# Attention in front of two expert stages: load order, the sink copy, four weight subtractions and the mask steps moved

## Chip, core and metric

The kernel runs on one core of a Trainium2 chip. The metric is the device time of one execution in microseconds. Two things have to be kept apart: the time of a run, and the span of one profiled execution, which is a little shorter than that execution's own time.

## What is computed

Inputs are `q`, `k`, `v` of shape (2, 8, 768, 64), batch by heads by tokens by head size. Three stages follow each other.

```python
scores = q @ k.T / sqrt(D)                       # per batch and head
keep = (key < n_sink) | ((row - key >= 0) & (row - key < window))   # n_sink 4, window 128
a = softmax(where(keep, scores, -1e9))
x = (a @ v)                                      # to 1536 tokens x 512
g = x @ w_gate;  x = (silu(g) * (x @ w_val)) @ w_out               # d_ff 1536
# then each token with skip_score > 0 goes to the one of 8 experts with the largest logit:
out = x + gate * relu(x @ w1[e]) @ w2[e]         # d_ff 1024
```

## The kernel before

**Attention.** The 1536 tokens are 12 tiles of 128 rows (`NT`), 6 for each batch (`QT`). Each tile has 4 pairs of heads (`HP`), so there are 48 pairs in all, numbered n. A row sees only its own tile, the tile before it and the sinks, so a tile other than the first of its batch has 208 score columns per head, of which 16 are a copy of the batch's first 16 keys, kept beside each key tile in `k_sb`. The first tile of a batch has 128 columns, and less work.

One list, `ORDER`, made by `attention_order()` (line 55), fixes the order of steps on TensorE, VectorE and ScalarE alike. It goes by groups g = 0, 2, 4, and so on. In group g each engine takes these steps, as far as they are its own:

- S for pairs g and g+1: TensorE makes scores (lines 1138 and 1145), VectorE adds the mask and finds the maximum (line 839), ScalarE takes the exponential (line 614)
- X for a finished tile: VectorE scales the tile's output into `xT` (line 862)
- T for pairs g-3 and g-2: TensorE transposes the probabilities (line 1166), VectorE (line 847) or, for the last pair of a tile, ScalarE (line 622) copies them from PSUM to `probsT`. With a tile's last pair goes Q: VectorE makes the reciprocals of the sums (lines 851 and 854)
- V for pairs g-5 and g-4: TensorE multiplies by the values (lines 1181, 1189). With a tile's last pair goes R: GpSimd spreads the reciprocals (line 526), TensorE transposes them (line 1159), ScalarE copies them (line 628)
- K, two mask steps on VectorE (`make_mask`, line 802, instructions of line 807). K for mask 1 comes right behind S of pair 2, K for mask 0 right behind S of pair 5 together with `find_wide` (lines 812 to 818). Mask 1 is first used in group 4, mask 0 in group 8
- W and M for the tiles in `EARLY` (7 to 10): at pair 1 of the tile ScalarE rounds a quarter of the next stage's first weights into `w_hi` (line 603); at pair 2, in the same group, VectorE subtracts to get `w_lo` (line 823)

TensorE's S of a group waits until the maxima of two groups of banks earlier are made (line 1134), and its second and later T until the copy of the T two before it is made (line 1155).

**Loads.** All of attention's loads are issued by SyncE (lines 358 to 382), in one queue: for each tile the columns of q and k (lines 367 and 368), then the values (lines 374 to 377). Columns of the second batch overwrite those of the first and wait for scores long made. From tile 3 on the values wait until the V steps of the tile three before are done (line 372), and everything issued later stands behind that wait. Between the tiles of batch 0 and those of batch 1 come five loads of weights (lines 380 to 382, 1554 KB together).

**GpSimd.** Its loop over tiles (lines 517 to 530) copies the sinks into the key tiles at tiles 0 and 6 (line 523), spreads the reciprocals of the tile, and then splits the tile before into `x_hi` and `x_lo` (lines 511 and 514). TensorE's first S of tiles 1 and 7 waits for the sink copy (line 1131).

**Behind attention** TensorE runs slices of the dense stage (lines 1198 to 1216): slice f needs 2f+2 halves of `w_lo`, its first chunk 8 split tiles, its last all 12. SyncE's next weight loads wait for `w_lo` too (line 399).

Of the kernel before, what the change touches and what calls it, by code (L numbers as in the profile page):

```python
# [7 lines left out]
F32 = mybir.dt.float32  # L8
# [6 lines left out]
P = 128  # L15
B, H, S, D = 2, 8, 768, 64
DM = H * D
QT = S // P
NT = B * QT
HP = H // 2  # L20
SK = 16
# [3 lines left out]
TAIL = SC - P  # L25
SINKS = slice(P, KT)
# [15 lines left out]
KB = 1024  # L42
PAIRS = NT * HP
EARLY = range(NT - 5, NT - 1)
MASK_AT = {2: 1, 5: 0}
TURNED = 4
WARM_UP = 24

# [6 lines left out]
def attention_order():  # L55

    steps, psum_use, turned = [], 0, {}  # L60
    for g in range(0, PAIRS + 10, 2):
        for n in (g, g + 1):
            if n < PAIRS:
                steps.append(("S", n // HP, n % HP, n))
                if n in MASK_AT:
                    steps.append(("K", MASK_AT[n], None, n))
        for n in (g - 7, g - 6):
            if 0 <= n < PAIRS and n % HP == HP - 1:
                steps.append(("X", n // HP, None, n // HP))
        for n in (g - 3, g - 2):  # L70
            if 0 <= n < PAIRS:
                steps.append(("T", n // HP, n % HP, psum_use))
                turned[psum_use] = n
                psum_use += 1
                if n % HP == HP - 1:
                    steps.append(("Q", n // HP, None, n // HP))
        for n in (g - 5, g - 4):
            if 0 <= n < PAIRS:
                tile, hp = divmod(n, HP)
                steps.append(("V", tile, hp, None))  # L80
                if hp == HP - 1:
                    steps.append(("R", tile, None, psum_use))
                    psum_use += 1
                if tile in EARLY and hp in (1, 2):
                    steps.append(("W" if hp == 1 else "M", tile, None, tile - EARLY[0]))
    v_use = itertools.count()
    return [(k, t, h, next(v_use)) if k == "V" else (k, t, h, n) for k, t, h, n in steps], turned

# [3 lines left out]
LAST_V = {tile: use for kind, tile, _, use in ORDER if kind == "V"}  # L92
# [10 lines left out]
def build(nc, qT, kT, v, va, vb, sizes, w_gv, w_out, w_route, w1, w2, out):  # L103
    ctx = ExitStack()
    with ctx:
# [17 lines left out]
        q_sb = place("q_sb", (P, HP, S), 0, 0)  # L123
        k_sb = place("k_sb", (P, HP, QT, KT), 0, 12)
# [231 lines left out]
        @block.sync  # L356
        def _(sp):
            sp.dma_start(sizes_i[:, :], sizes.broadcast_to([P, 4])).then_inc(sizes_in, 16)
            for b in range(B):
                for t in range(QT):  # L360
                    tok = slice(t * P, t * P + P)
                    if b:

                        sp.wait_ge(scores_ready, H * min(t + 2, QT))

                        sp.wait_ge(ksink_made, 1)
                    sp.dma_start(q_sb[:, :, tok], qT[b, :, :, tok]).then_inc(qk_in[t], 16)
                    sp.dma_start(k_sb[:, :, t, 0:P], kT[b, :, :, tok]).then_inc(qk_in[t], 16)
                    tile = b * QT + t
                    if tile >= 3:  # L370

                        sp.wait_ge(pv_done, LAST_V[tile - 3] + 1)
                    if t == 0:
                        sp.dma_start(va_sb[:, tile % 3, 0, :], v[b, 0, :, :]).then_inc(v_in[t], 16)
                    else:
                        sp.dma_start(va_sb[:, tile % 3, :, :], va[b, t - 1, :, :, :]).then_inc(v_in[t], 16)
                        sp.dma_start(vb_sb[0:TAIL, tile % 3, :, :], vb[b, t - 1, :, :, :]).then_inc(v_in[t], 16)
                if b == 0:
                    for f in range(2):
                        sp.dma_start(w_raw[:, f, :, :, :], w_gv[f, :, :, :, :]).then_inc(w_in[f], 16)  # L380
                        sp.dma_start(wo_raw[:, f, :], w_out[f, :, :]).then_inc(wo_in[f], 16)
                    sp.dma_start(wr_sb[:, :, :], w_route).then_inc(wr_in, 16)
# [83 lines left out]
        def _(pool):  # L466
# [41 lines left out]
            def split_x(tile):  # L508
                at_tok = slice(tile * P, tile * P + P)
                pool.wait_ge(o_ready, tile + 1)  # L510
                nc.gpsimd.tensor_copy(x_hi[:, :, at_tok], xT[:, tile % 2, :].rearrange("p (k t) -> p k t", k=KD)
                                      ).then_inc(x_hi_made, 1)
                pool.wait_ge(x_hi_made, tile + 1)
                nc.gpsimd.tensor_tensor(x_lo[:, :, at_tok], xT[:, tile % 2, :].rearrange("p (k t) -> p k t", k=KD),
                                        x_hi[:, :, at_tok].bitcast(F32), ALU.subtract).then_inc(xT_ready, 1)

            for tile in range(NT):
                if tile % QT == 0:

                    pool.wait_ge(qk_in[0], 32 * (tile // QT) + 32)  # L520
                    if tile:
                        pool.wait_ge(scores_ready, QT * H)
                    nc.gpsimd.tensor_copy(k_sb[:, :, 0:QT - 1, SINKS], k_sb[:, :, 0:1, 0:SK].broadcast_to(
                        [P, HP, QT - 1, SK])).then_inc(ksink_made, 1)
                pool.wait_ge(rsum_ready, tile + 1)
                nc.gpsimd.tensor_copy(rsum_wide.rearrange("p (h c) -> p h c", h=H),
                                      rsum[:, tile % 2, :].unsqueeze(2).broadcast_to([P, H, D])).then_inc(rsum_spread, 1)
                if tile:
                    split_x(tile - 1)
            split_x(NT - 1)  # L530

            with pool.Fori(0, FT1 // 2) as j:
# [234 lines left out]
        def _(d):  # L767
# [60 lines left out]
            for kind, tile, h, n in ORDER:  # L828
                qt = tile % QT
                if kind == "S":  # L830
                    cols = slice(0, SC if qt else P)
                    for u in range(2):
                        i = n * 2 + u
                        d.wait_ge(scores_ready, i + 1)
                        if i >= 4:

                            d.wait_ge(probs_ready, i - 3)

                        nc.vector.tensor_tensor_reduce(  # L839
                            out=scores_sb[:, i % 4, cols], in0=scores_ps[i % 4][:, cols],  # L840
                            in1=mask[:, max(2 - qt, 0), cols], scale=SCALE, scalar=3e38, op0=ALU.add, op1=ALU.min,
                            accum_out=negmax[:, i % 4:i % 4 + 1]).then_inc(max_ready, 1)
                elif kind == "T" and not on_act(kind, h):
                    d.wait_ge(pT_in_psum, n + 1)
                    if SBUF_USE[n] >= TURNED:
                        d.wait_ge(pv_done, SBUF_USE[n] - TURNED + 1)
                    nc.vector.tensor_copy(turned(probsT[:, SBUF_USE[n] % TURNED, :], qt), turned(pT_ps[n % 2][:, :], qt)
                                          ).then_inc(pT_by_dve, 1)
                elif kind == "Q":
                    d.wait_ge(probs_ready, tile * H + H)  # L850
                    nc.vector.tensor_scalar(rsum[:, tile % 2, :], sums[:, qt % 2, :], 1e-9, None, ALU.add
                                            ).then_inc(sums_step, 1)
                    d.wait_ge(sums_step, tile + 1)
                    nc.vector.reciprocal(rsum[:, tile % 2, :], rsum[:, tile % 2, :]).then_inc(rsum_ready, 1)
                elif kind == "X":
                    use = next(m for k, t, _, m in ORDER if k == "R" and t == tile)
                    d.wait_ge(pv_done, LAST_V[tile] + 1)
                    d.wait_ge(pT_by_act, evacuated(use)[1])
                    if tile >= 2:

                        d.wait_ge(xT_ready, tile - 1)
                    nc.vector.tensor_tensor(xT[:, tile % 2, :], o_ps[tile % 2][:, :], rbc_sb, ALU.mult
                                            ).then_inc(o_ready, 1)
                elif kind == "M":
                    split_half(n // 2, n % 2, n + 1)
                elif kind == "K":
                    make_mask(tile)
                    if tile == 0:
                        find_wide()
# [69 lines left out]
                        val_ps[(u + c) % 2][:, :].rearrange("p (t c) -> p t c", c=P), ALU.mult).then_inc(h_ready, 1)  # L939

            slice_of_h(0, 0)
            with d.Fori(0, FT1 // 2 - 1) as j:
                for u in (1, 0):
                    f = j * 2 + 2 - u
                    for half in range(2):
                        split_half(1 - u, half, (f + 1) * 2 + half + 1)
                    slice_of_h(f, u)
# [476 lines left out]
```

## Time and profile before

| | us |
|---|---|
| median of 3 runs | 592.85 |
| lowest, highest | 591.88, 593.5 |
| the profiled execution's own time | 595.78 |
| its span | 593.9 |
| attention within it, up to the dense stage's first product | 98.5 |

TensorE is busy for 548.1 us of the span, VectorE for 242.5, ScalarE for 180.7, GpSimd for 92.7. The span starts with the first instruction. The profile draws it in 40 slices of 14.85 us each; attention is the first six and a half. A slice shows busy time in tenths, and the clock that TensorE was granted, also in tenths: full speed is 2.4 GHz, half speed 1.2 GHz. TensorE's busy time is not work done: at half clock the same work is busy for longer.

### The profile page before, as it was taken

The page shows a single profiled execution, that of the slowest core. Times are in us where ns is not written, and L with a number is a line of the kernel's source. Part 1 is how long each engine was busy: PE and PEld are TensorE (multiplying, and loading weights), DVE is VectorE, ACT ScalarE, POOL GpSimd, SP SyncE. Part 2 cuts the span into 40 slices and gives each one's busy share as a digit, 9 for nine tenths or more (in the row PEclk, how much of TensorE's full clock was granted, in tenths as well). Part 3 has the DMA queues.
Part 4 walks back from the last instruction along what each step waited for, and adds up shares of the span by engine and source line. Part 5 has one row for each costly group of instructions (what it writes and reads, how often), then busy time and mean ns, then how long its engine had stood idle before and what let it go on. Part 6 is the DMA issues. An engine that isn't in the chain of part 4 may idle for free.

```text
span 593.9 us, 10567 instructions
## 1 busy us (share of the span) xinstructions
PE 548.1 (92%) x3752; PEld 462.9 (78%) x3752; DVE 242.5 (41%) x675; ACT 180.7 (30%) x419; POOL 92.7 (16%) x132
## 2 busy tenths in 40 slices
PE   6987889999999999999889999999269998999994
PEld 5766667788888888888768888888269997999993
DVE  6874774323333333232223344633624244145411
ACT  4764774110111111111123334321304133144210
POOL 2242335411111100100000110011100111102111
PEclk9997999999999999999979999999669999999998
DMA  8784750211111111000070112761455587755111
GB/s 224 216 266 110 216 157 4 73 53 53 53 53 53 53 53 53 0 0 1 0 284 35 53 53 76 279 230 58 156 172 218 196 313 300 307 212 190 59 36 35
DMA packets 29509, 73.55 MB, mean 124 GB/s; under 512 B 2816, under 2 KB 15104, under 8 KB 25376
## 3 DMA queue, kind: packets, MB, share of 16 engines
q1 hardware_dynamic: 26592, 63.61, 31.1%
q0 software_dynamic: 2880, 9.47, 4.7%
q8 instruction: 22, 0.36, 0.2%
q14 instruction: 15, 0.12, 0.1%
HBM read 61.77 MB, written 11.29 MB: 123 GB/s over the span
## 4 chain that ended last, share of the span: by engine, by line
PE 82%; DMA 7%; DVE 4%; ACT 3%; issue 3%; SPq 1%; POOL 0%; DVEq 0%; POOLq 0%; ACTq 0%
PE bank L1362 11%; PE bank L1203 11%; PE bank L1207 11%; PE bank L1205 11%; PE bank L1277 6%; PE bank L1281 5%; PE bank L1279 5%; PE bank L1374 3%; PE bank L1376 3%; PE bank L1375 3%; PE bank L1189 3%; DMA k_sb<-kT 2%; DMA w_raw<-w 2%; PE bank L1166 2%; PE bank L1145 2%
## 5 line engine op out<-in xcount | busy, mean ns | idle before, releaser
L1203 PE MATMUL bank<-x_hi,w_hi 128*128 128x512 f32 x288 | 112.2, 390 | 0.3 <-issue 0.3
L1207 PE MATMUL bank<-x_hi,w_lo 128*128 128x512 f32 x288 | 112.1, 389 | 0.0
L1205 PE MATMUL bank<-x_lo,w_hi 128*128 128x512 f32 x288 | 112.0, 389 | 0.0
L1362 PEld LDWEIGHTS bank<-xgT,w_sb 128*128 128x128 f32 x704 | 82.8, 197 | 1.9 <-issue 1.2
L1362 PE MATMUL bank<-xgT,w_sb 128*128 128x128 f32 x704 | 83.1, 280 | 0.8 <-ACT xgT L736 0.8
L934 DVE TENSOR_TENSOR sig<-sig,bank 128x512 f32<-128x512 f32 x36 | 24.8, 688 | 131.1 <-ACT sig L656 131.1
L656 ACT ACTIVATE sig<-bank 128x512 f32<-128x512 f32 x36 | 21.5, 599 | 162.6 <-PE bank L1207 162.6
L1277 PE MATMUL bank<-wo_hi,hh_hi 128*128 128x512 f32 x144 | 59.5, 414 | 4.3 <-DVE hh_lo L954 4.3
L1203 PEld LDWEIGHTS bank<-x_hi,w_hi 128*128 128x128 f32 x288 | 54.1, 188 | 11.8 <-issue 0.7
L1205 PEld LDWEIGHTS bank<-x_lo,w_hi 128*128 128x128 f32 x288 | 54.1, 188 | 11.3
L1207 PEld LDWEIGHTS bank<-x_hi,w_lo 128*128 128x128 f32 x288 | 54.0, 188 | 11.2
L1281 PE MATMUL bank<-wo_hi,hh_lo 128*128 128x512 f32 x144 | 57.4, 399 | 0.0
L1279 PE MATMUL bank<-wo_lo,hh_hi 128*128 128x512 f32 x144 | 57.2, 397 | 0.0
L1012 DVE TENSOR_TENSOR w_lo<-w_raw,w_hi 128x1024 fp32r<-128x1024 f32 x32 | 37.3, 1220 | 35.4 <-ACT w_hi L699 35.3
L614 ACT ACTIVATE probs<-scores_sb,negmax 128x208 f32<-128x208 f32 (+1 forms) x96 | 42.8, 448 | 28.1 <-DVE negmax L839 28.1
L699 ACT ACTIVATE w_hi<-w_raw 128x1024 fp32r<-128x1024 f32 x32 | 31.5, 1048 | 32.8 <-PE bank L1376 25.0
L549 POOL DMA_INDIRECT expert_rows<-x,row_i x12 | 11.8, 980 | 174.1 <-DVE row_i L1004 171.1
L839 DVE CUSTOM_DVE_ANT_0 scores_sb<-bank,mask 128x208 f32<-128x208 f32 (+1 forms) x96 | 28.9, 357 | 23.1 <-PE bank L1145 17.3
L1374 PE MATMUL bank<-w_hi,hg_hi 128*128 128x512 f32 x88 | 35.4, 402 | 2.1 <-DVE hg_lo L1092 2.1
L1277 PEld LDWEIGHTS bank<-wo_hi,hh_hi 128*128 128x128 f32 x144 | 27.7, 193 | 9.8 <-issue 4.7
L1376 PE MATMUL bank<-w_hi,hg_lo 128*128 128x512 f32 x88 | 34.4, 391 | 0.0
L1375 PE MATMUL bank<-w_lo,hg_hi 128*128 128x512 f32 x88 | 34.3, 390 | 0.0
(139 smaller groups left out, 692.9 us busy)
## 6 DMA issues: line engine op xcount, KB each, us to landing
w_sb<-w SPq DMA_DIRECT2D x16, 1024.0 KB, 6.2
w_raw<-w SPq DMA_DIRECT2D x16, 1024.0 KB, 9.4
w_raw<-w_gv SPq DMA_DIRECT2D x12, 512.0 KB, 3.6
va_sb<-v_long SPq DMA_DIRECT2D x10, 512.0 KB, 3.5
xg<-expert_rows POOLq DMA_DIRECT2D x13, 257.0 KB
vb_sb<-v_tail SPq DMA_DIRECT2D x10, 320.0 KB, 4.7
q_sb<-qT SPq DMA_DIRECT2D x12, 256.0 KB, 4.8
k_sb<-kT SPq DMA_DIRECT2D x12, 256.0 KB, 5.0
```

The lines of the kernel that those rows point to most:

```text
L614: nc.scalar.activation(probs[:, qt % 2, h * 2 + u, cols], scores_sb[:, i % 4, cols], ACT.Exp, bias=negmax[:, i % 4:i % 4 + 1], scale=-1.0, ...
L1012: last = nc.vector.tensor_tensor(w2_lo[u][:, f:f + FT2 // 4, :].rearrange("p k c -> p (k c)"), w2_raw[:, p, q:q + FT2 // 4, :].rearrange(" ...
L1203: nc.tensor.matmul(ps[:, :], w_hi[:, u, a, k, :], x_hi[:, k, tok], start=(k == 0), stop=False)
L1205: nc.tensor.matmul(ps[:, :], w_hi[:, u, a, k, :], x_lo[:, k, tok], start=False, stop=False)
L1207: last = nc.tensor.matmul(ps[:, :], w_lo[:, u, a, k, :], x_hi[:, k, tok], start=False, stop=(k == KD - 1))
L1277: nc.tensor.matmul(out_ps[u][:, :], hh_hi[:, u, f, :], wo_hi[:, f, :], start=(f == 0), stop=False, skip_group_check=True)
L1279: nc.tensor.matmul(out_ps[u][:, :], hh_hi[:, u, f, :], wo_lo[:, f, :], start=False, stop=False, skip_group_check=True)
L1281: last = nc.tensor.matmul(out_ps[u][:, :], hh_lo[:, u, f, :], wo_hi[:, f, :], start=False, stop=(f == FT1 - 1), skip_group_check=True)
L1362: last = nc.tensor.matmul(ps, w1_sb[u][:, k, fc], xgT[:, k * P:k * P + P], start=(k == 0), stop=(k == KD - 1))
L1374: nc.tensor.matmul(y_ps[:, :], hg_hi[:, hf], w2_hi[u % 2][:, f, :], start=(f == 0), stop=False)
L1375: nc.tensor.matmul(y_ps[:, :], hg_hi[:, hf], w2_lo[u % 2][:, f, :], start=False, stop=False)
L1376: last = nc.tensor.matmul(y_ps[:, :], hg_lo[:, hf], w2_hi[u % 2][:, f, :], start=False, stop=(f == FT2 - 1))
```

## The change

Four edits. The numbers of masks, copies, subtractions and loads stay the same.

1. SyncE issues the columns of tile t+1 before the values of tile t. The weights still follow the values of tile 5, but the columns of tile 6 are now ahead of them.
2. The second sink copy is asked for at tile 5 of GpSimd's loop, ahead of that tile's reciprocals, and no longer at tile 6.
3. Step M leaves the list. GpSimd makes the four subtractions (`split_w`), one behind each of its splits of tiles 7 to 10, and VectorE waits once for all four before its loop over slices.
4. The K steps move to the end of their groups, behind T and V: mask 1 to the end of group 2, mask 0 with `find_wide` to the end of group 6.

```diff
-MASK_AT = {2: 1, 5: 0}
+MASK_AT = {2: 1, 6: 0}
@@ attention_order
                 steps.append(("S", n // HP, n % HP, n))
-                if n in MASK_AT:
-                    steps.append(("K", MASK_AT[n], None, n))
...
-                if tile in EARLY and hp in (1, 2):
-                    steps.append(("W" if hp == 1 else "M", tile, None, tile - EARLY[0]))
+                if tile in EARLY and hp == 1:
+                    steps.append(("W", tile, None, tile - EARLY[0]))
+        if g in MASK_AT:
+            steps.append(("K", MASK_AT[g], None, g))
@@ sync
+            load_columns(0)
+            for tile in range(NT):
+                if tile + 1 < NT:
+                    load_columns(tile + 1)
+                load_values(tile)
+                if tile == QT - 1:
                     for f in range(2):
                         sp.dma_start(w_raw[:, f, :, :, :], w_gv[f, :, :, :, :]).then_inc(w_in[f], 16)
@@ gpsimd
+            def copy_sinks(b):
+                pool.wait_ge(qk_in[0], 32 * b + 32)
+                if b:
+                    pool.wait_ge(scores_ready, QT * H)
+                nc.gpsimd.tensor_copy(k_sb[:, :, 0:QT - 1, SINKS], k_sb[:, :, 0:1, 0:SK].broadcast_to(
+                    [P, HP, QT - 1, SK])).then_inc(ksink_made, 1)
+
+            def split_w(n):
+                u, half = divmod(n, 2)
+                pool.wait_ge(w_hi_made, n + 1)
+                nc.gpsimd.tensor_tensor(w_lo[:, u, half, :, :], w_raw[:, u, half, :, :],
+                                        w_hi[:, u, half, :, :].bitcast(F32), ALU.subtract).then_inc(w_lo_made, 1)
+
+            copy_sinks(0)
             for tile in range(NT):
-                if tile % QT == 0:
...
+                if tile == QT - 1:
+                    copy_sinks(1)
                 pool.wait_ge(rsum_ready, tile + 1)
...
                 if tile:
                     split_x(tile - 1)
+                    if tile - 1 in EARLY:
+                        split_w(tile - 1 - EARLY[0])
@@ vector
-                elif kind == "M":
-                    split_half(n // 2, n % 2, n + 1)
...
             slice_of_h(0, 0)
+            d.wait_ge(w_lo_made, len(EARLY))
```

## Rows read from the trace of the kernel before

**Rows 1.** The page: busy share of TensorE and its granted clock, 40 slices.
```profile
PE   6987889999999999999889999999269998999994
PEclk9997999999999999999979999999669999999998
```

**Rows 2.** Busy time by stretch: stretch, us, busy (instructions) by engine, clock, DMA, GB/s.
```profile
6.50:19.66 13.16, 9.84 (x121) 6.55 (x120) 10.95 (x65) 9.73 (x42) 0.61 (x1) 1.00 0.94 243
19.66:26.39 6.73, 6.73 (x121) 5.22 (x117) 5.18 (x22) 4.92 (x19) 2.45 (x3) 1.00 0.73 208
39.84:44.87 5.03, 3.04 (x61) 2.36 (x57) 2.71 (x12) 2.49 (x10) 2.07 (x3) 1.00 0.98 310
44.87:49.83 4.96, 4.96 (x52) 3.95 (x52) 2.23 (x10) 2.25 (x9) 0.37 (x1) 0.66 0.23 62
55.28:59.73 4.45, 4.45 (x45) 3.04 (x45) 1.93 (x10) 2.44 (x9) 0.00 (x0) 0.62 0.12 18
61.99:66.23 4.24, 3.67 (x54) 2.58 (x54) 3.48 (x14) 3.50 (x14) 2.46 (x3) 1.00 0.68 160
66.23:73.97 7.74, 6.75 (x121) 5.22 (x123) 5.78 (x23) 5.44 (x20) 2.87 (x3) 1.00 0.69 210
sum 92.20, PE 79.89 PEld 60.71 DVE 63.52 ACT 59.01 POOL 28.61; mean PE 5.71 PEld 4.34 DVE 4.54 ACT 4.22 POOL 2.04
```

**Rows 3.** Instructions in time order around tile 6's first scores: start, us, engine, line.
```profile
31.97 0.33 SPq L376 DMA_DIRECT2D va_sb<-v_long  x1
37.00 0.79 SPq L368 DMA_DIRECT2D k_sb<-kT  x1
44.87 0.72 PE L1138 MATMUL bank<-k_sb,q_sb 64*128 64x128 f32 x8 [1.99 <-DMA k_sb<-kT]
```

**Rows 4.** Time order around tile 7's first scores.
```profile
54.73 0.45 POOL L523 COPY k_sb<-k_sb 128x320 f32<-128x320 f32 x1
55.28 0.93 PE L1145 MATMUL bank<-k_sb,q_sb 64*64 64x208 f32 x16 [2.84 <-issue]
```

**Rows 5.** Chain of waits: two full-clock pieces, and the same two after the first wait.
```profile
20.60 1.02 PE bank L1166 x8
25.20 0.64 PE bank L1159 x4
...
45.59 1.34 PE bank L1166 x8
47.98 1.05 PE bank L1159 x4
```

**Rows 6.** Time order around the first of the four W and M steps.
```profile
69.52 0.62 ACT L603 ACTIVATE w_hi<-w_raw 128x512 fp32r<-128x512 f32 x1
70.17 0.69 DVE L823 TENSOR_TENSOR w_lo<-w_raw,w_hi 128x512 fp32r<-128x512 f32 x1 [0.62 <-ACT w_hi L603]
70.30 1.70 POOL L514 TENSOR_TENSOR x_lo<-xT,x_hi 128x512 fp32r<-128x512 f32 x1
72.70 0.66 PE L1159 MATMUL bank<-ident,rsum_wide 128*128 128x128 f32 x4 [0.99 <-DVE probsT L847]
```

**Rows 7.** Time order: an `x_lo` subtraction where VectorE made no `w_lo`.
```profile
63.89 1.28 POOL L514 TENSOR_TENSOR x_lo<-xT,x_hi 128x512 fp32r<-128x512 f32 x1
```

**Rows 8.** Time order at the start of attention: masks, copies, scores.
```profile
10.19 0.94 PE L1145 MATMUL bank<-k_sb,q_sb 64*64 64x208 f32 x16 [1.09 <-DMA k_sb<-kT]
12.01 0.82 DVE L807 TENSOR_SCALAR mask<-keep 64x128 bf16<-64x128 f32 x6
13.71 0.74 DVE L847 COPY probsT<-bank 128x256 f32<-128x256 f32 x2
14.18 0.99 PE L1166 MATMUL bank<-ident,probs 128*128 128x128 f32 x6 [1.24 <-DVE probsT L847]
19.05 0.31 PEld L1189 LDWEIGHTS bank<-probsT,va_sb 128*64 128x64 f32 x8 [0.17 <-DVE probsT L847]
20.30 0.38 DVE L839 CUSTOM_DVE_ANT_0 scores_sb<-bank,mask 128x208 f32<-128x208 f32 x1 [1.29 <-PE bank L1145]
```

More of the change, by code:

```diff
@@ L358, in _, with load_columns, load_values @@
             sp.dma_start(sizes_i[:, :], sizes.broadcast_to([P, 4])).then_inc(sizes_in, 16)
[L359 to L378, printed above, removed]
+            def load_columns(tile):
+                b, t = divmod(tile, QT)
+                tok = slice(t * P, t * P + P)
+                if b:
+                    sp.wait_ge(scores_ready, H * min(t + 2, QT))
+                    sp.wait_ge(ksink_made, 1)
+                sp.dma_start(q_sb[:, :, tok], qT[b, :, :, tok]).then_inc(qk_in[t], 16)
+                sp.dma_start(k_sb[:, :, t, 0:P], kT[b, :, :, tok]).then_inc(qk_in[t], 16)
+            def load_values(tile):
+                b, t = divmod(tile, QT)
+                if tile >= 3:
+                    sp.wait_ge(pv_done, LAST_V[tile - 3] + 1)
+                if t == 0:
+                    sp.dma_start(va_sb[:, tile % 3, 0, :], v[b, 0, :, :]).then_inc(v_in[t], 16)
+                else:
+                    sp.dma_start(va_sb[:, tile % 3, :, :], va[b, t - 1, :, :, :]).then_inc(v_in[t], 16)
+                    sp.dma_start(vb_sb[0:TAIL, tile % 3, :, :], vb[b, t - 1, :, :, :]).then_inc(v_in[t], 16)
+            load_columns(0)
[4 more added lines that the diff above has]
+                if tile == QT - 1:
                     for f in range(2):
@@ L515, in split_x @@
                                         x_hi[:, :, at_tok].bitcast(F32), ALU.subtract).then_inc(xT_ready, 1)
-            for tile in range(NT):
-                if tile % QT == 0:
[L520 to L524, printed above, removed]
+            def copy_sinks(b):
+                pool.wait_ge(qk_in[0], 32 * b + 32)
+                if b:
+                    pool.wait_ge(scores_ready, QT * H)
[7 more added lines that the diff above has]
+            copy_sinks(0)
+            for tile in range(NT):
+                if tile == QT - 1:
+                    copy_sinks(1)
                 pool.wait_ge(rsum_ready, tile + 1)
```

## Prediction

> **What bounds the kernel now.** I read the page first. TensorE is busy in nine tenths or more of most slices, and all four edits lie in attention, where it is not: its digits are 6, 9, 8, 7, 8, 8 and the clock digit falls to 7 once, in the fourth slice [rows 1]. So the question is what TensorE waits for in attention, and how much of that the edits remove; behind it the dense stage is busy back to back and starts when attention ends.
>
> The second view is busy time by stretch. I cut attention from 6.5 to 98.7 us at the starts of score groups. Of 92.20 us TensorE is busy for 79.89, so 12.31 are waits (the sum line of [rows 2]). A tile in the middle of batch 0 takes 6.73 us with no wait at all; that is the floor of a full tile (the second line of [rows 2]). Against it stand five kinds of loss:
> - the start, 6.50 to 19.66: 13.16 - 9.84 = 3.32 us
> - tile 6's first scores: 5.03 - 3.04 = 1.99 us
> - tile 7's first scores: 2.84 us [rows 4]
> - 61.99 to 66.23: 4.24 - 3.67 = 0.57 us
> - the three stretches of 7.7 us from 66.23 on, of which one is shown: 7.74 - 6.75 = 0.99 each, 2.97 together, and 0.6 in the last stretch.
>
> A sixth loss hides in the busy time. Behind each of the two long waits the granted clock is low: 0.66 and 0.62 over stretches of 4.96 and 4.45 us, against 1.00 in the others [rows 2]. That is the level of 1.2 GHz for most of the stretch. The chain of waits gives its price: eight transposes take 1.34 us there and 1.02 at full clock, four of line 1159 take 1.05 and 0.64 [rows 5].
>
> **Edit 1, columns ahead.** The wait before 44.87 is for the k columns of tile 6 [rows 3]. They were issued at 37.00 behind the values of tile 5 (31.97) and five weight loads, and took until 44.8, 7.8 us, to land. After the change they stand right behind the values of tile 4, one tile (6.7 us) before 31.97, so at about 26; with no weights ahead even the same 7.8 us would have them in by 34, nine before they are asked for. The wait of 1.99 us goes. What is late next? The columns of tile 7 take the place of tile 6's behind the weights: issued at about 37, landed at 44.8 at the latest. They are first used one tile 6 later, at 42.9 + 3.5 + 2.6 = 49.0 us on the old scale, less what the start gains (below): still some 2.5 us in hand. The values of each tile keep their wait on the tile three before; in the steady part they are the first thing issued when it opens, in both kernels. At the very start `v` of tile 0 moves behind the columns of tile 1, and `va`, `vb` of tile 1 behind those of tile 2; with 512 KB ahead at the stretch's 243 GB/s [rows 2] that is some 2 us later. They landed at 13.4 and are first used at 19.05 [rows 8]. Cost nothing.
>
> The clock goes with the wait. At full clock the pieces of group 24 are 0.72 + 1.02 + 0.61 + 0.64 + 0.62 = 3.61 us; they took 0.72 + 1.34 + 1.05 + 1.05 + 0.87 = 5.03. **1.42 us.** The two pieces shown [rows 5] carry 0.73 of it.
>
> **Edit 2, the sink copy.** The 2.84 us before 55.28 are put down to "issue", but GpSimd tells the cause [rows 4]. The copy of line 523 runs at 54.73, ends at 55.18, and TensorE starts at 55.28. In GpSimd's program it stands behind the spread of tile 5's reciprocals and the split of tile 4. After the change it is asked for when the split of tile 3 is done and scores of tile 5 are made: both hold by 45.3 us on the old scale (the last `x_lo` before it runs at 43.97 for 1.26 us). That is over 3 us before TensorE wants it, and the reciprocals of tile 5 need scores of tile 5 anyway, so the new wait in front of them costs nothing; only the copy's own 0.45 us lies there, on an engine that idles for 4 to 7 us a tile. **2.84 us.** The low clock behind it goes with it: at full clock that group's pieces are shorter by 0.07 + 0.35 + 0.44 + 0.41 + 0.26 = **1.5 us**.
>
> Both together: 1.99 + 1.42 + 2.84 + 1.5 = 7.75 us.
>
> **Edit 3, M to GpSimd.** In a group with W and M, VectorE stands still for 0.62 us until ScalarE's `w_hi` is done, then works 0.69 on `w_lo`, and only then takes the next scores [rows 6]. The scores give ScalarE its exponentials late and the copies late, and TensorE's transposes of line 1159 wait 0.99 us for VectorE's copy [rows 6]. The stretch with M has 0.99 us of wait, one without has none. With M gone VectorE is free at 69.55 instead of 70.86, TensorE's scores are there at about 69.8, and ScalarE, which keeps W, is free at 70.14, about when the first maximum arrives (70.1). So the whole 0.99 goes in three stretches: 2.97 us. In the fourth the tail of attention follows; VectorE's copies there started at 93.98 for transposes whose first half was ready near 93.4. I take **0.5 us**. Together 3.5 us; the low end is 2.5, if W still delays ScalarE by some 0.3 a tile, as its idle time there is no more than W's own 0.62.
>
> On GpSimd each tile now has 0.56 + 0.70 + 1.28 + one subtraction. The nearest row of its price is `x_lo`, of the same size and type: 1.28 us, 1.70 at worst [rows 6 and 7]. That makes 3.8 to 4.6 us of a tile of 6.73. What is queued behind it is the next tile's spread, and for that TensorE waits; the spread is ready 3.0 us before TensorE takes it, and what TensorE waits for at 72.70 is VectorE's copy [rows 6]. The `w_hi` it waits for is four groups old by then. At the end the fourth subtraction stands before the split of tile 11, which ended at 102.2 and is asked for by the third chunk, about 11 us after 98.5: 7 us in hand. SyncE's weight loads for slice 2 wait for the second `w_lo`, now half a tile to a tile later, but are wanted 30 us on. Cost nothing.
>
> The Trainium skill (SBUF — State Buffer, section SBUF: two separate sides) says that VectorE, when it has two SBUF inputs or runs in a two-port mode, and GpSimd take one pair of ports by turns, whole instructions long. The trace leans that way: `x_lo` beside `w_lo` took 1.70 us, alone 1.28 [rows 6, 7]. By the rule the move is good for GpSimd here; against it, the mask step, now beside GpSimd's first spread of 0.61 us, could be held for that long. The sum would be 0.6 us less by it.
>
> **Edit 4, masks.** Now VectorE makes mask 0 and `find_wide` from 12.01 to 13.7, between the scores of group 4 and the copies of T that TensorE needs; TensorE waits 1.24 us for them [rows 8]. VectorE is the bound of this start: 10.95 us of 13.16 busy. Walked through with the durations of the trace: columns of tile 1 land about 1 us sooner, since 256 KB of values no longer stand ahead (they are waited for 1.09 us [rows 8]); mask 1 falls into the gap that this leaves. Scores of group 4 are then done at 11.6 instead of 12.0, the copies at 12.4 instead of 14.45, and mask 0 runs from 14.5 to 16.3, while TensorE has group 8's transposes and values to do, which are 3 us. VectorE then goes straight on to its copies, until 18.8, and finds group 10's scores waiting, where before it idled 1.29 us up to 20.30 [rows 8]. That is 1.5 us gained on VectorE, and near 2 on TensorE once VectorE has caught up (it works 5.18 us of each 6.73). I take **1.6 us**. From below 0, if the mask before group 8's scores only holds the next group instead; from above 3.3, all of the start's waits.
>
> **The sum.** 7.75 + 3.5 + 1.6 = 12.8 us. Check against the ceiling: all waits and the lost clock are 12.31 + 2.9 = 15.2. The profiled execution had a span of 593.9 and a time of 595.78; a stretch shortened within it shortens both alike. The median of the runs is 2.9 lower than that time, and none of the edits touches what lies between, so I take the sum off the median: 592.85 - 12.8 = **580.0 us** (off the profiled time, 583.0).
>
> **Rivals.**
> - **The clock does not come back.** Tiles 6 and 7 are light and TensorE may still meet a wait there, as it does from 61.99 to 66.23 [rows 2]. Against it: that stretch has 0.57 us of waits at clock 1.00, and the start has one of 1.24 at full clock. Then 2.9 us stay: 582.9. Chance 0.13.
> - **The wait moves from tile 6 to tile 7.** Its columns now stand behind the weights. If they or the next values land late, a wait of 2.0 us with its clock, 1.4, comes back: 3.4 us, 583.4. Against it: 2.5 us in hand. Chance 0.08.
> - **VectorE keeps the start.** Mask 0 sits before group 8's scores and all TensorE gains is paid there: 1.6 less, with W's 1.0 on ScalarE 2.6 less: 581.6 to 582.6. Chance 0.15.
> - **More than forecast.** The start gives 3.3 and the tail its 0.6: 578.2, and the ceiling 577.7. Chance 0.10.
> - **Slower: GpSimd becomes the bound.** If its subtraction of `w` took time D, its work per tile is 2.54 + D. Above D = 4.2 it passes 6.73, and TensorE's line 1159 waits for the spread in four tiles. To eat the other 12.8 us and end later than before it needs 4 (D - 4.2) over 12.8, so D over 7.4 us; at 8 us the time is 592.85 - 12.8 + 15.2 = 595.3. The same kind of instruction takes 1.28 to 1.70. Chance 0.01.
> - **The change does nothing measurable:** the waits named are not what held TensorE, and others as long stand behind them: 592.9. Chance 0.01. Each wait has its releaser within 0.1 us of its end, and no other engine is near its bound there.
>
> **How the numbers follow.** The forecast's own case has 0.52, with 579 to 581.5. The range 577.7 to 584.0 takes in the ceiling, both bounds of edits 3 and 4 and the first three rivals, each with the 0.6 us by which the runs scatter; less than two in ten is outside. A measurement of this kernel can tell about 0.3%, 1.8 us, from no change, and all cases but the last two are over 8 us faster: faster 0.98, same 0.01, slower 0.01.
>
> **What would show it.** Right: in the changed kernel TensorE has no wait over 1 us between 20 and 90 us, the clock is 1.00 throughout attention, tiles 7 to 10 take 6.73 us each, the sink copy runs more than 2 us before tile 7's first scores, and the dense stage's first product starts near 85.7 us instead of 98.5. Wrong: a low clock digit in the fourth or a neighbouring slice, a wait for `k_sb` or values anywhere after 20 us, waits of TensorE for `rsum_wide`, or a dense stage that has grown by what attention gave.

## The result and the profile after

The changed kernel takes 585.41 us, median of four runs (585.08 to 586.5), against 593.16 of the kernel before beside it: ratio 0.9876 (95% interval 0.9856 to 0.9897), or 7.4 us less, 6.1 to 8.5. A second series of six runs gave 586.11 against 593.88, ratio 0.9873 (0.9842 to 0.9904). The forecast was 580.0, with a range from 577.7 to 584.0. The kernel is faster, but by some 5 us less than the sum said.

The profiled execution took 585.22 us, with a span of 583.3. These lines are from its page: busy time by engine, then TensorE's busy share and granted clock in 40 slices of 14.6 us.

```profile
PE 546.4 (94%) x3752; PEld 461.8 (79%) x3752; DVE 240.3 (41%) x671; ACT 180.7 (31%) x419; POOL 95.3 (16%) x136
...
PE   7899999999999999999799999999189998999994
...
PEclk9999999999999999999889999999579999999998
```

The dip of the clock in the fourth slice [rows 1] is gone, and TensorE's busy share reads 9 from the third slice to the end of attention, where it fell to 7 and 8 before. The dense stage starts at 88.92 us, not 98.47; from there to the end it is 494.4 us, before 495.4 (in the other profiles below it lies between 493.1 and 495.3, whatever the kernel). So the gain is made in attention. By stretches of the changed kernel (columns as in [rows 2]):

```profile
7.72:21.02 13.30, 10.44 (x121) 6.77 (x120) 11.05 (x65) 9.63 (x42) 0.61 (x1) 1.00 1.09 294
41.21:44.17 2.96, 2.96 (x60) 2.35 (x56) 2.30 (x12) 2.00 (x10) 0.08 (x1) 1.00 1.12 329
44.17:47.66 3.49, 3.49 (x57) 2.87 (x53) 2.55 (x11) 2.64 (x11) 2.74 (x4) 1.00 0.56 145
50.19:53.44 3.25, 3.09 (x48) 2.10 (x45) 2.08 (x11) 2.64 (x10) 2.34 (x3) 1.00 0.73 176
59.85:66.58 6.73, 6.73 (x120) 5.23 (x117) 5.18 (x22) 5.44 (x20) 2.44 (x3) 1.00 0.74 200
80.04:88.92 8.88, 8.42 (x160) 6.99 (x157) 4.98 (x17) 4.20 (x13) 4.88 (x7) 1.00 0.18 61
```

Each of these lines has its fellow in [rows 2]. The group in front of tile 6 takes 2.96 us where it took 5.03, its follower 3.49 for 4.96, tile 7's first group 3.25 for 4.45, and a tile with W 6.73 for 7.74. Only the first line has not shrunk: the start, from the first scores of all to those of pair 10, takes 13.30 us, where the same stretch took 13.14 (6.52 to 19.66). And it begins at 7.72, not at 6.52, because the warm-up ahead of it (24 transposes that TensorE makes while the first columns are loaded) took longer.

GpSimd's part in time order: the sink copy ends 3.2 us ahead of tile 7's first scores (50.19), and a subtraction of `w` costs what one of `x` costs.

```profile
46.55 0.44 POOL L531 COPY k_sb<-k_sb 128x320 f32<-128x320 f32 x1
...
70.71 1.28 POOL L523 TENSOR_TENSOR x_lo<-xT,x_hi 128x512 fp32r<-128x512 f32 x1
71.95 1.27 POOL L537 TENSOR_TENSOR w_lo<-w_raw,w_hi 128x512 fp32r<-128x512 f32 x1
```

The start of the changed kernel holds the one wait that was not there before. In time order, from group 8's scores (L1165) over the mask (L828) and VectorE's scores and copies (L860, L868) to TensorE's transposes of the reciprocals (L1179):

```profile
15.50 0.93 PE L1165 MATMUL bank<-k_sb,q_sb 64*64 64x208 f32 x16
16.09 0.86 DVE L828 TENSOR_SCALAR mask<-keep 64x128 bf16<-64x128 f32 x6
...
17.90 0.38 DVE L860 CUSTOM_DVE_ANT_0 scores_sb<-bank,mask 128x208 f32<-128x208 f32 x1
...
19.08 1.28 DVE L868 COPY probsT<-bank 128x512 f32<-128x512 f32 x2
19.82 0.66 PE L1179 MATMUL bank<-ident,rsum_wide 128*128 128x128 f32 x4 [1.68 <-DVE probsT L868]
...
21.66 0.38 DVE L860 CUSTOM_DVE_ANT_0 scores_sb<-bank,mask 128x208 f32<-128x208 f32 x1 [1.29 <-PE bank L1165]
```

Group 8's scores start at 15.50, 7.78 us behind the first of all; before it was 9.17. Then the lead is lost: TensorE stands for 1.68 us. Transposes write to two PSUM banks by turns, so the bank of R (the transposes of the reciprocals) is free only when VectorE has copied the T two before it, and that copy stands behind four scores, and they behind mask 0 and `find_wide`. The last line shows VectorE idle for 1.29 us ahead of group 10's scores, exactly as before [rows 8].

### The profile page after: what moved, and what is told of

Its sections match the earlier page's. It is cut to its first block, busy times and chain, and to the rows that moved or that the text cites. A ratio compares the mean times of both kernels' runs of the same rounds, so it can differ in the third digit from the quotient of the medians.

```text
span 583.3 us, 10567 instructions
## 1 busy us (share of the span) xinstructions
PE 546.4 (94%) x3752; PEld 461.8 (79%) x3752; DVE 240.3 (41%) x671; ACT 180.7 (31%) x419; POOL 95.3 (16%) x136
## 4 chain that ended last, share of the span: by engine, by line
PE 88%; DVE 4%; DMA 4%; issue 2%; ACT 1%; POOL 0%; DVEq 0%; POOLq 0%; ACTq 0%
PE bank L1382 12%; PE bank L1223 11%; PE bank L1225 11%; PE bank L1227 11%; PE bank L1297 6%; PE bank L1301 6%; PE bank L1299 6%; PE bank L1209 4%; PE bank L1394 3%; PE bank L1396 3%; PE bank L1395 3%; PE bank L1186 3%; PE bank L1165 2%; DMA w_raw<-w 2%; PE bank L1317 1%
## 5 line engine op out<-in xcount | busy, mean ns | idle before, releaser
L1223 PEld LDWEIGHTS bank<-x_hi,w_hi 128*128 128x128 f32 x288 | 54.1, 188 | 11.9 <-issue 0.8
L860 DVE CUSTOM_DVE_ANT_0 scores_sb<-bank,mask 128x208 f32<-128x208 f32 (+1 forms) x96 | 29.0, 357 | 17.4 <-PE bank L1165 13.4
L763 ACT ACTIVATE hg_hi<-bank 128x512 fp32r<-128x512 f32 x22 | 13.0, 593 | 70.0 <-PE bank L1382 70.0
```

Of the source, the lines that this page charges most:

```text
L1223: nc.tensor.matmul(ps[:, :], w_hi[:, u, a, k, :], x_hi[:, k, tok], start=(k == 0), stop=False)
```

## Experiments

Each kernel was timed against the kernel before on the same chip; of the kernel before, two more single executions were profiled. Differences in microseconds are one minus the ratio, times 593.4. The kernels were not all timed on one chip, so they are compared with each other by these differences.

**Other profiles of the kernel before.** The profile on which the prediction rests was of an execution of 595.78 us, above all three runs shown. Does each execution lose what that one lost?

> The kernel before once more, for a second profile of it. Theory A (chance at the start): how fast the 24 warm-up transposes of line 1125 go differs from run to run whatever the kernel; they took 4.17 us in the first profile of before and 5.38 in that of the changed kernel, and in this one they take anything between 4.1 and 5.4. Theory B (the change slows them): they take 4.2 us again. Of the clock: the first profile of before was 2.9 us above the median of the runs. If the low clock behind the two long waits is there in each run, the stretches 44.87 to 49.83 and 55.28 to 59.73 take 4.96 and 4.45 us again; if it comes and goes, one of them is near 3.6 or 3.0 and the run is nearer to 593.

> The kernel before, a third profile. So far a wait of 2.8 us on TensorE was followed by a low clock in three profiles of five (before, its second look and edit 3 alone had it; masks alone and edit 1 alone did not). Theory A (a matter of chance in each execution): the stretch behind tile 7's first scores takes either 3.25 or 4.5 us here, and the wait for tile 6's columns is 0.9 to 1.5 us, at full clock behind it. Theory B (each execution of this kernel pays for both waits): 4.5 us, and a wait of 2.0 with a stretch of 4.96 behind it.

They took 592.86 and 593.44 us. Stretches of the first of them: the group in front of tile 6, its follower, and tile 7's first group.

```profile
39.60:43.60 4.00, 3.04 (x60) 2.36 (x57) 2.71 (x12) 2.48 (x10) 1.12 (x2) 1.00 1.12 325
43.60:47.09 3.49, 3.49 (x53) 2.88 (x53) 2.13 (x10) 2.16 (x9) 1.31 (x2) 1.00 0.23 44
...
52.52:57.04 4.52, 4.51 (x45) 3.13 (x45) 2.03 (x10) 2.18 (x9) 0.00 (x0) 0.62 0.03 10
```

The wait for tile 6's columns is 4.00 - 3.04 = 1.0 us, not 2.0, and the clock behind it stays at 1.00: 3.49 us where the first profile had 4.96. Behind the second wait the clock is low here as there. The second has 1.4 us for the first wait, 3.48 behind it, and 4.51 behind the second. So theory A holds for the first wait: with the profiles below it is 0.9 to 2.0 us from execution to execution, and of what the first profile paid for it (1.99 + 1.42) the others pay a third or so. Of the second wait these two profiles decide nothing: 4.5 us fits both theories.

The warm-up took 4.17, 4.24 and 4.86 us in the three profiles of the kernel before, and 5.38 in both of the changed one; the kernels below show 4.52 to 5.38. The 4.24 alone fitted theory B; the 4.86, and 5.38 with edit 2 alone, make it theory A. The first scores start as the warm-up ends.

**Edit 1 alone.** The diff is that of SyncE's program.

> Edit 1 alone: columns of the next tile ahead of the values, all else as before. Two looks at the kernel before disagree on what the wait for tile 6's columns takes: 2.0 us with a low clock behind it in the one, 1.0 us at full clock in the other. Theory A (the second is the common case): 1.0 to 1.5 us faster than before. Theory B (the first is): 3.4 us faster. Both: no wait for k_sb after 20 us, and the wait of 2.8 us before tile 7's scores stays.

591.91 us, ratio 0.997 (0.9942 to 0.9998): 1.8 us faster, 0.1 to 3.4. No wait for `k_sb` is left in its list of waits, and tile 7's wait stays. The clock behind it, over the same group:

```profile
51.64:54.88 3.24, 3.09 (x45) 2.15 (x45) 1.93 (x10) 2.18 (x9) 0.00 (x0) 1.00 0.04 14
```

It takes 3.24 us at full clock, behind the same wait of 2.83 us that led to 4.5 in others. Theory A fits, theory B is at the edge of the interval.

**Edit 2 alone.** The diff is the move of `copy_sinks(1)`.

> Edit 2 alone: the second sink copy ahead of tile 5's reciprocals. Both theories: the wait of 2.84 us before tile 7's first scores goes whole, since the copy runs more than 2 us before them. Theory A (the low clock behind that wait is there in about half of the executions, and costs 1.3 us where it is): 2.8 to 4.1 us faster, near 3.5. Theory B (it is there in each): 4.3 us faster. A result under 2.5 would say that another wait takes its place.

588.85 us, ratio 0.9931 (0.9905 to 0.9956): 4.1 us faster, 2.6 to 5.6. The copy ran at 45.99, tile 7's scores at 51.03 with no wait. Groups 26 and 28 of this kernel:

```profile
48.50:51.03 2.53, 2.53 (x51) 2.17 (x47) 1.98 (x12) 1.76 (x10) 0.10 (x1) 1.00 0.96 323
51.03:54.27 3.24, 3.09 (x48) 2.10 (x44) 2.07 (x11) 2.63 (x10) 2.35 (x3) 1.00 0.68 177
```

The whole 2.84 is gone, and so is what the clock cost, 4.51 - 3.24 = 1.27 where it was paid; together 4.1. The interval holds both theories.

**Edit 3 alone.** The diff takes M out of the list and adds `split_w`.

> Edit 3 alone: the four subtractions on GpSimd. Theory A (three stretches of 7.74 us become 6.73, and the tail gains 0.2): 3.2 us faster. Theory B (as forecast): 3.5 us. Theory C (GpSimd's queue delays the spreads or ScalarE's W keeps part of the wait): 2.5 us or less. The stretches from group 34 to group 46 take 20.2 us in all by A and B, against 23.2 before.

590.42 us, ratio 0.9963 (0.9942 to 0.9984): 2.2 us faster, 1.0 to 3.4. The first two of its three tiles with W, and the tail:

```profile
64.37:71.10 6.73, 6.73 (x121) 5.22 (x117) 5.18 (x22) 5.44 (x20) 2.44 (x3) 1.00 0.68 196
71.10:77.82 6.72, 6.72 (x120) 5.22 (x116) 5.18 (x22) 5.42 (x20) 3.68 (x4) 1.00 0.75 208
...
84.55:93.44 8.89, 8.43 (x161) 7.00 (x157) 4.97 (x17) 4.20 (x13) 4.89 (x7) 1.00 0.18 61
```

The stretch from group 34 to 46 is 20.18 us where it was 23.21, 3.0 less, as by A and B. The tail gains 9.10 - 8.89 = 0.2, not the 0.5 of B. By the trace, then, it is A, with 3.2 us. The runs say a little less, and their interval would also hold the 2.5 of C; but the stretches and the waits of the trace leave no room for C.

**Edit 4 alone.** The diff is that of `MASK_AT` and of the place of K.

> Edit 4 alone: the mask steps at the end of groups 2 and 6, all else as before. Theory A (a missed link): TensorE's transposes of line 1159 in group 8 need VectorE's copies, which now stand behind the masks and the scores; a wait of about 1.7 us appears there and eats what the earlier groups gain. Time equal to before within 0.7 us, first scores of tile 3 (group 12) at 22.7 +-0.5 plus what the warm-up takes longer. Theory B (as forecast, hidden by a slow start of one profile): 1.0 to 1.6 us faster than before, no wait over 0.6 us in group 8.

595.03 us, ratio 1.0026 (1.0003 to 1.0049): 1.5 us slower, 0.2 to 2.9, not faster, so theory B is out. Its trace has the wait of the changed kernel, as theory A said. The second line is tile 7's first group:

```profile
19.84 0.66 PE L1159 MATMUL bank<-ident,rsum_wide 128*128 128x128 f32 x4 [1.69 <-DVE probsT L847]
...
54.05:57.28 3.23, 3.09 (x44) 2.14 (x45) 1.93 (x10) 2.18 (x9) 0.00 (x0) 1.00 0.05 15
```

From the first scores of all to those of group 12 it takes 16.28 us. The kernel before takes 16.11, 15.80 and 15.63 in its three profiles, the changed one 16.27 and 16.04. That makes 0.3 to 0.5 us of loss which the traces show. The rest of the 1.5 is not seen in this one, and it can hardly be: it is of the fastest of the kernel's twelve executions, 592.28 us, 2.8 below their median. It had the wait of 2.8 us before tile 7 and no low clock behind it, 3.23 us. The profile of edit 1 alone, the other without the low clock, was 2.0 below its median too (589.92 for 591.91); the four with it were 0.7 below to 2.9 above. So a median execution may well have paid the 1.27 us.

**Edits 1 to 3 without 4.**

> Edits 1, 2 and 3 without edit 4 (masks where they were before). Theory A (edit 4 gives nothing or costs): as fast as the changed kernel or up to 1.5 us faster, 7.7 to 9.2 us faster than before. Theory B (edit 4 gives 1.6 as forecast): 1.6 us slower than the changed kernel, so about 6 us faster than before.

583.7 us, ratio 0.9843 (0.9815 to 0.9871): 9.3 us faster than before, 1.8 more than the changed kernel's 7.5, though the intervals overlap. Its start takes 15.63 us to group 12. That is theory A; B's 6 us lies outside the interval.

**The wait in group 8.** To show that VectorE's queue ahead of group 8's copies is what TensorE pays for, `find_wide` alone was taken out of it and put at the end of group 8, where VectorE idled.

```diff
+        if g == 8:
+            steps.append(("F", 0, None, g))
...
                     make_mask(tile)
-                    if tile == 0:
-                        find_wide()
+                elif kind == "F":
+                    find_wide()
```

> All four edits, but find_wide (five small steps, 0.85 us on VectorE) moves on from the end of group 6 to the end of group 8. Theory A (what VectorE does in front of group 8's scores is paid one for one by TensorE): the wait of 1.68 us for VectorE's copy shrinks to about 0.8 and the kernel is 0.8 us faster than the changed one. Theory B (the start is not set by VectorE's queue): no change.

583.26 us, ratio 0.9824 (0.9797 to 0.9852): 10.4 us faster than before. The wait is 0.9 us shorter, by just the 0.9 us of `find_wide`, and VectorE's idle time ahead of group 10's scores is 0.44 us where it was 1.29:

```profile
18.25 0.66 PE L1181 MATMUL bank<-ident,rsum_wide 128*128 128x128 f32 x4 [0.78 <-DVE probsT L870]
...
20.08 0.37 DVE L862 CUSTOM_DVE_ANT_0 scores_sb<-bank,mask 128x208 f32<-128x208 f32 x1 [0.44 <-PE bank L1167]
```

The start takes 15.07 us, 1.2 less than in the changed kernel in its first profile and 1.0 less than in its second. Of that, 0.9 is the wait; the rest is that the first eight scores took 1.01 and 0.78 us there and 0.71 here. So it is theory A. By the runs the kernel is 2.9 to 3.0 us faster than the changed one, more than the trace accounts for; the intervals leave room for less, and why it may be more is not known.

**`find_wide` at the end of group 14, mask 0 at the end of group 4** (`MASK_AT = {2: 1, 4: 0}`, `if g == 14`).

> Edits 1 to 3, with mask 0 at the end of group 4 (behind its copies, before any scores of group 6) and find_wide out of the start, at the end of group 14, where VectorE idles 1.3 us per group pair. Theory A (TensorE pays for each microsecond that VectorE's queue holds between group 4's scores and group 8's copies): no wait over 0.8 us for VectorE's copies in the first 20 us, first scores of group 12 at most 15.0 us behind the first scores of all, against 15.1 with late find_wide, 15.6 with the old mask places, 16.3 in the changed kernel; 1.3 us faster than the changed kernel, 0.6 faster than with the old mask places. Theory B (the landing of the columns sets the start): no gain over the old places.

588.41 us, ratio 0.9928 (0.9902 to 0.9954): 4.3 us faster than before, far less than expected. The start is nearly as expected, 15.16 us. The rest is not, and the expectation had the place wrong: VectorE's idle 1.3 us [rows 8] come before the scores of group 10, so behind group 8's work, once a tile; the end of group 14 is the other place, in front of a group with R. In time order:

```profile
30.19 0.51 DVE L838 TENSOR_TENSOR wide_f<-few 128x1 f32<-128x1 f32 x1
30.73 0.16 DVE L839 SCALAR_TENSOR_TENSOR wide_f<-lim,wide_f 128x1 f32<-128x1 f32 x1
30.77 1.27 POOL L525 TENSOR_TENSOR x_lo<-xT,x_hi 128x512 fp32r<-128x512 f32 x1
30.93 1.13 DVE L840 SCALAR_TENSOR_TENSOR wide_f<-lim,wide_f 128x1 f32<-128x1 f32 x1
...
34.13 0.66 PE L1181 MATMUL bank<-ident,rsum_wide 128*128 128x128 f32 x4 [1.95 <-DVE probsT L870]
```

The five steps took 2.3 us, not 0.85, because two of them ran beside GpSimd's splits (see the last section). TensorE waited 1.95 us, and the group behind ran with a low clock, 4.42 us for 2.97:

```profile
35.45:39.87 4.42, 4.42 (x59) 3.28 (x57) 2.93 (x12) 2.40 (x9) 1.05 (x2) 0.65 0.96 304
```

2.08 us in group 16 and 1.45 behind it make 3.5 us, most of what parts this kernel from the next.

**Mask 0 at the end of group 4, `find_wide` at the end of group 8.**

> Late find_wide (end of group 8), and mask 0 at the end of group 4 in place of group 6. Theory A (in group 8 TensorE waits for VectorE's copies, and only what VectorE does between group 8's scores and those copies or just ahead of them counts): the wait of 0.8 us in group 8 shrinks to below 0.3, but mask 0 now holds the scores of group 6, so that the kernel is 0 to 0.6 us faster than with mask 0 at group 6. The run with find_wide at the end of group 14 showed a wait of 2.0 us and a low clock in group 16; at group 8 neither appears, and this kernel is about 4 us faster than that one.

584.77 us, ratio 0.9843 (0.9812 to 0.9874): 9.3 us faster than before, 5.0 more than with `find_wide` at group 14, where about 4 were expected. With mask 0 at group 6 it was 10.4, so the 0 to 0.6 us that its earlier place was to give did not come. The wait in group 8 is gone from its list, but the start takes 15.14 us, as with mask 0 at group 6. So in the two places tried the mask's 0.87 us is paid, in group 6 or in group 8; only `find_wide` was to be had for nothing.

**A shorter warm-up**, over late `find_wide`.

```diff
-WARM_UP = 24
+WARM_UP = 16
```

> Late find_wide (end of group 8), with 16 warm-up transposes in place of 24. In all profiles TensorE's first scores start when the warm-up ends (6.5 to 7.7 us), while their columns are in at 5.7. Theory A (the warm-up holds the first scores): they start near 6.0, and the kernel is 0.5 to 1.5 us faster than with 24. Theory B (without the full warm-up the first scores run at the low clock): they start near 6.0 but the first group takes 1.2 us where it took 0.7, and nothing is gained.

581.39 us, ratio 0.9799 (0.9765 to 0.9832): 11.9 us faster than before. In time order, warm-up and first scores:

```profile
2.41 3.67 PE L1147 MATMUL bank<-ident 128*128 128x128 f32 x16 [2.41 <-POOL ident L484]
6.02 1.23 PE L1160 MATMUL bank<-k_sb,q_sb 64*128 64x128 f32 x8
```

The first scores start at 6.02, not 7.35, and take 1.23 us, not 0.71; the start to group 12 is 15.38 for 15.07. Of 1.3 us gained some 1.0 is left in the trace: A, less a part of B. The granted clock reads 1.00 in both profiles here, so B's cause, a low clock, is not shown. By the runs the kernel is 1.5 us faster than with 24 transposes; that fits, but the two intervals overlap. It is the lowest ratio of the study.

**The changed kernel again.**

> The changed kernel once more, timed against the kernel before with as many runs as the parts. By the parts measured alone (1.8 for the columns, 4.1 for the sink copy, 2.2 to 3.0 for the subtractions, minus 1.5 for the masks) it is 6.6 to 7.5 us faster than before; by the forecast 12.8.

586.11 us, 7.5 us faster than before. The parts alone add up to 1.8 + 4.1 + 2.2 - 1.5 = 6.6. Within their scatter, which is 1 to 2 us for each part, they explain the whole; an effect of one on another is not needed, though one of a microsecond or two could hide in it.

## Why the prediction was wrong where it was

**Right.** What TensorE waits for and what frees it: both long waits went, with the time that they had (2.84, and whatever the columns' was). Nothing took their place: tile 7's columns behind the weights were not waited for. The three tiles with W fell from 7.7 to 6.73 us, each. GpSimd's subtraction costs 1.27 us as its neighbour row said, and its spread came in time. The columns of tile 1 came 0.85 us sooner. Behind 20 us none of the rivals' waits appeared.

**The step that failed: edit 4.** It was to give 1.6 us and costs 0.3 to 0.5 by the traces, 1.5 in the runs with it alone. The walk sent TensorE through "group 8's transposes and values", 3 us of work, while VectorE made the mask, and then had group 10's scores waiting for VectorE. It left out that R, between those values, takes the bank of the T two before it (the wait of line 1155, which the text ahead names for T alone, is one of R too), and so waits for a copy that VectorE makes behind the mask, `find_wide` and four scores. The text was near the truth for VectorE: "from 14.5 to 16.3" for mask 0 with `find_wide` and "until 18.8" for the copies, where the trace has 14.9 to 16.7 and 19.2, once the 1.2 us of later start are taken off. What it drew from them for TensorE was wrong: group 10 cannot start before R and the values behind it, so VectorE idles its 1.29 us ahead of group 10 as before, and no time is gained. VectorE had been the bound of the start, and moving its work within its queue moves the wait. Late `find_wide` shows it: 0.9 us less queue, 0.9 us less wait. The sign that the text listed, no wait over 1 us between 20 and 90 us, could not show it: this wait ends at 19.82.

**Terms that were mis-sized.** Edit 1's 1.99 and 1.42 us, and edit 2's 1.5 for the clock. They were read from one profile of one execution that was 2.9 us above the median, and taken off the median. Against that very profile they came out: the stretches from group 10 to group 30 are 7.65 us shorter, where 7.75 were forecast (1.5 for the second clock was a little too much, 4.45 - 3.25 = 1.2). But the other profiles put the columns' wait at 0.9 to 1.5 us, with full clock behind. Behind the 2.8 us wait the clock was low in four of six profiles that have it (the kernel before three times, edit 3 alone; not with edit 4 alone nor edit 1 alone), at 1.27 us: 0.8 on the mean, and up to 1.27 if the median execution pays it each time. Edits 1 and 2 then come to 1.2 + 2.84 + 0.8 to 1.27, so 4.8 to 5.3 us, where 7.75 were taken; measured alone, 1.8 + 4.1. The tail gave 0.2, not 0.5.

With 3.2 for edit 3 and 0.4 lost by edit 4, the traces make 7.6 to 8.1 us, against 7.4 and 7.5 measured and 12.8 forecast. With the 1.5 that edit 4 lost in the runs it is 6.5 to 7.0. This sum was made afterwards, so it shows that the sizes fit, not that each is right. By it, the forecast was too high by 2.5 to 3 us in these two waits and their clock, by 2.0 in edit 4 (3.1 by the runs), and by 0.3 in the tail.

The dense stage was to start near 85.7 and started at 88.92. Of these 3.2 us, 1.2 are the longer warm-up, 1.8 the start (0.16 lost for 1.6 gained), and 0.3 the tail.

**The sign of the profile's own excess.** The prediction said that no edit touches what lies between the profiled execution's time and the median. Edit 1 did: some 2 of those 2.9 us, the long form of the first wait and the clock behind it (1.99 + 1.42 for 1.2), were in the sum. Such an excess should have been a low end for the terms that can vary.

**The rivals.** "VectorE keeps the start" named the mechanism and priced it at zero gain. It was the nearest in its mechanism, but it had no room for a loss, though the text's own low bound was "from below 0". The clock's rival asked the wrong question: not whether a low clock stays, but whether it was there to be removed.

**The page on ports.** By the rule of the Trainium skill (SBUF — State Buffer, section SBUF: two separate sides) the mask beside GpSimd's spread might be held for 0.6 us. It was not: mask 0 began at 16.09 beside a spread of 15.67 to 16.28 and took 0.86 us against 0.82. These steps have one SBUF input.

**What stays open.** Why edit 4 alone costs 1.5 us in the runs and 0.3 to 0.5 in the traces. The warm-up took its longest, 5.38 us, in all three profiles with edit 4 as it stands, but also in two without it or with other places (edit 2 alone, `find_wide` at group 14), and TensorE's program up to there is the same; whether the edit has a part in it was not told apart. The granted clock reads 1.00 throughout the warm-up in the profiles at 4.17 and at 5.38 us alike, so it does not tell why one is slower.

## What to carry to other kernels

When work is moved within the queue of an engine that sets the pace, walk every reader of that queue forward, bank by bank, and not only the next one: a step pays where the first result behind it is needed, and the free place is where that engine idles. Before a wait's length and the clock behind it are put into a sum, ask how the profiled execution stands to the median; if it is above it, the parts that can vary carry the excess. Here two more profiles of the old kernel would have moved the forecast by some 2.5 us.

## What the hardware showed

- **TensorE's clock behind a wait is not the same in each execution.** Behind waits of 0.9 to 1.7 us it stayed at full speed each time, behind one of 1.95 and one of 1.99 it was low, behind 2.8 it was low in four of six. At the lower level (1.2 GHz for most of a group) a group cost 1.3 to 1.5 us more.
- **The warm-up's speed varies too:** 24 transposes took from 4.17 to 5.38 us. Where the first work waits for the warm-up and not for its data (in at 5.7 us), attention starts up to 1.2 us later.
- **Even the smallest VectorE step with two SBUF inputs can be held up by GpSimd.** With `find_wide` at the end of group 14, a step of one element per partition took 1.13 us and ended at 32.06, with GpSimd's subtraction that had started before it (30.77 to 32.04); in the changed kernel, with GpSimd idle, the same step takes 0.16. Another took 0.51 for 0.16 and ended at 30.70, with a cast of GpSimd (30.08 to 30.69). The Trainium skill (SBUF — State Buffer, section SBUF: two separate sides) says that such a step and a GpSimd step that reads SBUF hold the shared ports by turns, for whole instructions; the trace agrees with it to 0.02 us in both.
